# A delta-rule attention with masked copies of its diagonal blocks, a shorter norm, and the first batch of the following FFT mixing begun inside the attention's last steps

## What is computed

```python
# batch 4, 8 heads, 768 tokens, head size 48
k_n = k / (np.linalg.norm(k, axis=-1, keepdims=True) + 1e-06)
for t in range(S):
    y[:, :, t] = einsum('bhd,bhde->bhe', q[:, :, t], state)
    v_old = einsum('bhde,bhd->bhe', state, k_n[:, :, t])
    state = state + bt * einsum('bhd,bhe->bhde', k_n[:, :, t], v[:, :, t] - v_old)

# mixing, on x of 4 x 768 x 384 (the heads side by side)
mixed = np.real(np.fft.fft(np.fft.fft(x, axis=1), axis=2))
u = x + mixed
un = (u - mean(u)) / np.sqrt(var(u) + 1e-06)
x = u + np.maximum(un @ w_ch1, 0.0) @ w_ch2
```

## Time and profile before

| | |
|---|---|
| median of 3 runs | 904.81 us (901.88 to 904.92) |
| profiled execution, own time | 899.3 us |
| its span | 897.5 us |
| TensorE busy | 834.6 us (93%) |
| VectorE busy | 475.1 us (53%) |
| ScalarE busy | 301.3 us (34%) |
| GpSimd busy | 199.4 us (22%) |
| chain that ended last: TensorE, issue, VectorE, ScalarE | 61%, 20%, 11%, 4% |

### The profile page before, as it was taken

One profiled execution on the slowest core, in us unless ns is written; L12 is line 12 of the kernel. 1 busy time (PEld: TensorE's weight loads), 2 busy tenths in 40 slices (PEclk: granted clock), 3 DMA queues, 4 the chain that ended last, 5 costly groups with the idle time before them and its releaser, 6 DMA issues.

```text
span 897.5 us, 24703 instructions
## 1 busy us (share of the span) xinstructions
PE 834.6 (93%) x10634; PEld 809.9 (90%) x10634; DVE 475.1 (53%) x1092; ACT 301.3 (34%) x654; POOL 199.4 (22%) x167
## 2 busy tenths in 40 slices
PE   7368999999984999999999999999999999999998
PEld 6368989899884999999999999999899899899898
DVE  5999999999295554435443443333632432432421
ACT  4246575675431221122111211123441431431421
POOL 3123123023001803600540000000132222222231
PEclk9758779697886999999999999999999999999999
DMA  6633454422564030012000103003410010000001
GB/s 198 163 121 99 148 148 119 132 58 74 158 215 131 3 123 19 18 54 70 18 18 14 56 18 116 20 15 105 152 53 27 27 53 27 26 0 27 27 1 53
DMA packets 38074, 65.14 MB, mean 73 GB/s; under 512 B 4249, under 2 KB 26082, under 8 KB 37986
## 3 DMA queue, kind: packets, MB, share of 16 engines
q1 hardware_dynamic: 37986, 63.85, 22.7%
HBM read 46.86 MB, written 14.16 MB: 68 GB/s over the span
## 4 chain that ended last, share of the span: by engine, by line
PE 61%; issue 20%; DVE 11%; ACT 4%; POOL 2%; DMA 1%; SPq 1%; POOLq 0%; ACTq 0%; DVEq 0%
PE m_ps_h L1111 13%; PE g_ps_v L1622 11%; PE m_ps_d L1111 11%; PE ps_ga L423 4%; PE g_ps_y L1622 3%; PE g_ps_u L1622 3%; PE ps_y L509 3%; PE ps_y L514 2%; PE ps_u L492 2%; DVE t_lane L603 2%; DVE prod L599 2%; PE ps_r L474 2%; ACT tt L346 2%; PE ps_s L527 2%; POOL g_vn_lo L1519 2%
## 5 line engine op out<-in xcount | busy, mean ns | idle before, releaser
L1111 PE MATMUL m_ps_h<-m_unt_hi,m_w_hi 128*128 128x256 f32 x432 | 122.7, 284 | 2.1 <-DVE m_unt_lo L1301 2.1
L1111 PE MATMUL m_ps_h<-m_unt_lo,m_w_hi 128*128 128x256 f32 x432 | 121.9, 282 | 0.0
L1111 PE MATMUL m_ps_h<-m_unt_hi,m_w_lo 128*128 128x256 f32 x432 | 121.8, 282 | 0.0
L1307 DVE SCALAR_TENSOR_TENSOR m_h_lo<-m_ps_h,m_h_hi 128x512 fp32r<-128x512 f32 x72 | 49.8, 692 | 107.8 <-ACT m_h_hi L1011 107.8
L1111 PE MATMUL m_ps_d<-m_w_hi,m_h_hi 128*128 128x384 f32 x288 | 97.6, 339 | 0.0
L1111 PE MATMUL m_ps_d<-m_w_hi,m_h_lo 128*128 128x384 f32 x288 | 96.4, 335 | 0.0
L1111 PE MATMUL m_ps_d<-m_w_lo,m_h_hi 128*128 128x384 f32 x288 | 96.3, 334 | 0.0
L1011 ACT ACTIVATE m_h_hi<-m_ps_h 128x512 fp32r<-128x512 f32 x72 | 43.1, 598 | 151.0 <-PE m_ps_h L1111 151.0
L1111 PEld LDWEIGHTS m_ps_h<-m_unt_hi,m_w_hi 128*128 128x128 f32 x432 | 82.4, 191 | 2.6 <-DVE m_unt_lo L1301 2.5
L1111 PEld LDWEIGHTS m_ps_h<-m_unt_hi,m_w_lo 128*128 128x128 f32 x432 | 83.5, 193 | 0.0
L1111 PEld LDWEIGHTS m_ps_h<-m_unt_lo,m_w_hi 128*128 128x128 f32 x432 | 82.5, 191 | 0.0
(11 more groups left out here) (220 smaller groups left out, 1963.5 us busy)
## 6 DMA issues: line engine op xcount, KB each, us to landing
kq<-kq_g SPq DMA_DIRECT2D x48, 256.0 KB, 3.6
v_in<-v_g SPq DMA_DIRECT2D x12, 384.0 KB, 4.2
k_in<-k_g SPq DMA_DIRECT2D x12, 384.0 KB, 3.6
x_scr<-y_sb SPq DMA_DIRECT2D x24, 192.0 KB, 2.9
stage<-w_ch SPq DMA_DIRECT2D x6, 768.0 KB, 4.8
x_scr<-m_x_sb SPq DMA_DIRECT2D x24, 192.0 KB, 1.9
g_x<-x_scr SPq DMA_DIRECT2D x24, 192.0 KB, 4.5
out<-g_y SPq DMA_DIRECT2D x24, 192.0 KB, 1.9
```

The costliest lines, as they stand in the source:

```text
L1111: last = pe.matmul(out, first[x], second[y], start=(k == 0 and m == 0), stop=(k == n - 1 and m == 2))
L1307: dve.scalar_tensor_tensor(h_lo[:, 2 * g:2 * g + 2].rearrange("p f t -> p (f t)"), ps_h[g % 2][:, :], 0.0, h_hi[:, 2 * g:2 * g + 2].rearra ...
```

## The change

In the attention:

- `kmax` is gone; the root takes the diagonal of `g_lane` itself, with scale 0.25 and a small bias, so it is half the norm, and the Newton step then takes two operations where it took three. The last product of `lanes` is written straight into the diagonal of `t_lane`, which saves a copy; scaling `g_lane` now waits for it.
- `corners(g, c)` copies for one half of the units on all 128 partitions, twice, each time multiplied by a column of `half` that is 1 on the partitions wanted and 0 on the others. So `tt` needs no clearing at the start. Half c = 0 comes before the group, half c = 1 in its step 1, and `ps_u` waits only for the half it uses. Group 0 is now ordered like the others.
- The four Gram pieces of a group move by one step: from n = 4 to 7 to n = 5, 6, 7 and, for the last, step 0 of the next group (`gram_at`). Fetching them (`diagonal`) moves with them.
- The Gram pieces of group 2 wait until count 46 of group 0's chain.

In the mixing:

- The half of the first batch's spectrum that needs only early rows is multiplied inside the attention: cosines in step 5 and sines in step 6 of the last group. The sums lie in the banks `ps_e`, `ps_o` and `ps_d` until the second half is added.
- The early pieces of `x_tok` are loaded in steps 3 and 4 of the last group, the late ones straight from `y_sb`, not from DRAM.
- Chunk 2 of the weights is rounded on ScalarE, its remainder taken after `spectrum`; chunks 3, 4 and 5 have their remainders taken in `hidden(0, 0)`, behind g = 0, 2 and 4 (before: chunk 3 in `split` ahead of the spectrum, chunk 4 behind `norm`, chunk 5 behind g = 2).

```diff
+    def gram_at(i, n):
+        if n >= 5 and i + 3 < G:
+            return i + 3, n - 5
+        return (i + 2, 3) if n == 0 and i and i + 2 < G else None
...
             def roots(g):
-                act.wait_ge(kmax_ok, g + 1)
-                act.activation(root[:], kmax[:, g % 2], ACT.Sqrt).then_inc(root_ok, 1)
+                act.wait_ge(glane_ok, g + 1)
+                act.activation(root[:], ksum(g), ACT.Sqrt, bias=tiny[:, 0:1], scale=0.25).then_inc(root_ok, 1)
...
-                for a in (2 * h, 2 * h + 1):
-                    last = act.activation(tt[g % 2][quarter(a), :, H * (a % 2):H * (a % 2) + H], t_cols[quarter(a)],
-                                          ACT.Copy)
+                for a in range(2):
+                    last = act.activation(tt[g % 2][:, us, H * a:H * a + H], t_cols[:, us], ACT.Identity,
+                                          scale=half[:, a:a + 1])
                 last.then_inc(corner_ok, 1)
...
                 if 0 < i < G - 1 and n == 0:
                     solved_x(i, 0)
-                    corners(i, 1)
...
-                if 0 < i < G - 1 and n == 1:
+                if i < G - 1 and n == 1:
                     solved_w(i, 1)
+                    corners(i, 1)
...
             for what, g in FIRST:
+                if (what, g) == ("g", 2):
+                    pe.wait_ge(chain, WARM)
...
                     if m % NB == 0:
-                        pe.wait_ge(corner_ok, 2 * (g + 1))
+                        pe.wait_ge(corner_ok, 2 * g + c + 1)
...
+                for products in ahead.get(k - N * (G - 1), ()):
+                    products(pe)
...
-                dve.tensor_tensor(quot[:], ksum(g), rinv[:], ALU.mult).then_inc(newton, 1)
+                dve.scalar_tensor_tensor(quot[:], ksum(g), 0.25, rinv[:], ALU.mult, ALU.mult).then_inc(newton, 1)
                 link(2)
-                dve.tensor_tensor(quot[:], quot[:], root[:], ALU.add).then_inc(newton, 1)
+                dve.scalar_tensor_tensor(norm_l[:], quot[:], 1e-6, root[:], ALU.add, ALU.add).then_inc(newton, 1)
                 link(3)
-                dve.tensor_scalar(norm_l[:], quot[:], 0.5, 1e-6, ALU.mult, ALU.add).then_inc(newton, 1)
...
+        def residual_ahead(sp, first, last):
+            sp.wait_ge(att["ga_done"], att["pieces"] - 1)
+            rows = x_scr[0].rearrange("(m o) d -> o m d", o=2)
+            for part, t, k in early[first:last]:
+                m = k // 2
+                sp.dma_start(x_tok[part, t], rows[k % 2, m:m + part.stop - part.start]).then_inc(xt_in, 16)
...
+        def first_spectrum(pe, q, even, odd, n):
+            x, tab, m = (x_sin, ts_sb, MS) if q else (x_cos, tc_sb, MC)
+            pe.wait_ge(tab_in, 32)
+            pe.wait_ge(sin_ok if q else cos_ok, n + 1)
+            for ps, tiles in ((odd, (1, 3)), (even, (0, 2))):
+                for c in range(2):
+                    last = pe.matmul(ps[0:m, NK * c:NK * c + NK], x[:, c, tiles[n]], tab[:, tiles[n]],
+                                     start=(n == 0 and c == 0), stop=(n == 1), skip_group_check=True)
...
-                    if first and g == 2:
-                        weights(WC - 1)
+                    if first and g % 2 == 0:
+                        weights(DT + g // 2)
...
-            split(DT)
             spectrum(0, 0, ps_e, True)
-            spectrum(0, 1, ps_h[0], True)
+            spectrum(0, 1, ps_d[0], True)
+            weights(DT - 1)
             sums(0, 0)
             mirror(0, 0)
             norm(0, 0)
-            weights(NS)
```

More of the change, by code:

```diff
@@ L98, in attention @@
         beta = sb("beta", [P, G, H])
-        kmax = sb("kmax", [P, 2, H])
+        half = sb("half", [P, 2])
+        tiny = sb("tiny", [P, 1])
         root, rinv, quot, norm_l, rn, scale = (
@@ L260, in clear @@
                 pool.memset(t_lane[:], 0.0).then_inc(tl_zero, 1)
+            pool.memset(tiny[:], TINY / 4).then_inc(half_ok, 1)
+            pool.memset(half[:], 0.0).then_inc(half_ok, 1)
+            pool.wait_ge(half_ok, 2)
+            for a in range(4):
+                pool.memset(half[quarter(a), a % 2:a % 2 + 1], 1.0).then_inc(half_ok, 1)
+            pool.wait_ge(half_ok, 6)
             pool.memset(tri[:], 1.0).then_inc(tri_ok, 1)
@@ L276, in gpsimd @@
                                pattern=[[-1, P]], channel_multiplier=1).then_inc(ident_ok, 1)
-            for p in range(2):
-                pool.memset(tt[p][:], 0.0).then_inc(tt_zero, 1)
-            pool.wait_ge(tt_zero, 2)
             pool.wait_ge(ident_ok, 2)
@@ L534, in tensor @@
                     piece("a", i + 1, n - 2)
-                if n >= 4 and i + 3 < G:
-                    piece("g", i + 3, n - 4)
-                if i and n == 1:
+                if gram_at(i, n):
+                    piece("g", *gram_at(i, n))
+                if n == 1:
                     couple_w(i, 1)
-                if i and n == 2:
+                if n == 2:
                     couple_x(i, 1)
@@ L631, in last_inverse @@
                 dve.wait_ge(u_done, N * (g - 1))
-                for a in range(4):
-                    part = dve.tensor_copy(tt[g % 2][quarter(a), :, H * (a % 2):H * (a % 2) + H], t_cols[quarter(a)])
-                    if a % 2:
-                        part.then_inc(corner_ok, 1)
                 for c in range(2):
                     us = slice(HU * c, HU * c + HU)
+                    for a in range(2):
+                        part = dve.tensor_scalar(tt[g % 2][:, us, H * a:H * a + H], t_cols[:, us], half[:, a:a + 1], None,
+                                                 ALU.mult)
+                    part.then_inc(corner_ok, 1)
                     m = turn["w", g, c]
@@ L680, in upward @@
 def upward(tile, S):
+    end = S // 2 + P
     pieces = []
     for part, k, step in tokens(tile, S):
-        pieces.append((part, k if k < S // 2 else S + S // 2 - 1 - k))
+        row = k if k < S // 2 else S + S // 2 - 1 - k
+        n = (end - row + 1) // 2
+        if S // 2 <= row < end and part.start + n < part.stop:
+            pieces += [(slice(part.start, part.start + n), row), (slice(part.start + n, part.stop), row + 2 * n)]
+        else:
+            pieces.append((part, row))
     return pieces
@@ L872, in weights_ahead @@
             load_weights(sp, c)
+        first_tokens = [(part, t, k) for t in range(TT) for part, k in upward(t, S)]
+        late = [piece for piece in first_tokens if HS <= piece[2] < HS + P]
+        early = [piece for piece in first_tokens if piece not in late]
+        def residual_ahead(sp, first, last):
[4 more added lines that the diff above has]
+                sp.dma_start(x_tok[part, t], rows[k % 2, m:m + part.stop - part.start]).then_inc(xt_in, 16)
         ahead = {-2: (tables_ahead,), -1: (lambda sp: tokens_ahead(sp, 0, 3),), 0: (lambda sp: tokens_ahead(sp, 3, XE - 2),),
-                 1: (lambda sp: tokens_ahead(sp, XE - 2, XE),)}
-        for c in range(NS):
-            ahead[2 + c] = (lambda sp, c=c: weights_ahead(sp, c),)
+                 1: (lambda sp: tokens_ahead(sp, XE - 2, XE),), 2: (lambda sp: weights_ahead(sp, 0),),
+                 3: (lambda sp: weights_ahead(sp, 1), lambda sp: residual_ahead(sp, 0, len(early) // 2)),
+                 4: (lambda sp: weights_ahead(sp, 2), lambda sp: residual_ahead(sp, len(early) // 2, len(early)))}
         def first_batch(sp, results):
@@ L882, in first_batch @@
             sp.dma_start(x_in_sb[0:ROWS[3], 1, 3], results[0:P:2]).then_inc(x_in, 16)
+            for part, t, k in late:
+                sp.dma_start(x_tok[part, t], results[k - HS:P:2]).then_inc(xt_in, 16)
+            weights_ahead(sp, DT)
         def later_weights(sp):
@@ L1040, in batch @@
                     ahead["hi"](act, 0, ahead["split"])
+            act.wait_ge(att["ga_done"], att["pieces"])
+            act.wait_ge(att["corner_ok"], 2 * last_group + 2)
+            act.wait_ge(w_lo, DT - 1)
+            weights(DT - 1)
             odd_part(0, 0, ps_o, True)
-            odd_part(0, 1, ps_h[1], True)
+            odd_part(0, 1, ps_d[1], True)
+            act.wait_ge(att["y_done"], att["steps"])
+            weights(DT)
             for q in att["y_out"]:
@@ L1188, in first_weights_split @@
                 dve.wait_ge(att["corner_ok"], 2 * last_group + 2)
-                for c in range(DT):
+                for c in range(DT - 1):
                     split(c)
```

114 lines of the change are left out of this document (55 added, 59 removed).

## The result

| | before | after |
|---|---|---|
| median | 904.03 us (899.17 to 905.65) | 895.3 us (892.17 to 900.33) |
| profiled execution, own time | 899.3 us | 894.69 us |
| its span | 897.5 us | 892.9 us |

The ratio of the two is 0.992, with a 95% interval of 0.9899 to 0.9942: faster by 0.8%, 7 us, where 16.5 had been forecast; the median lies 2.3 us above the forecast's 884 to 893, within the wider range of 879 to 896.

A forecast was written before the change was run, and what follows sets the result against it. Bounds: VectorE's chain of inverses and the recurrence on TensorE and ScalarE in the attention, then the first batch's late residual. 11.5 + 6.5 - 1.5 = 16.5 us off 904.8 gave 888.3; forecast 884 to 893, wider range 879 to 896.

The forecast's parts named there:

- The norms: VectorE's chain in the attention: dropping kmax, a Newton operation and a copy saves about 0.1 us a group, 0.5 in group 0.
- The chain's floor: VectorE's chain of inverses: t_rows of group 5 starts at 214.7 us if no chain is held up.
- The recurrence: Group 2 on TensorE and ScalarE: 1152 matmuls, 31.9 us, plus 2 for the passage, 34 us where it took 40.2.
- the passage: Change from one attention group to the next, where TensorE waited and its clock fell: 2 us put on top of the matmuls.
- The attention: Whole attention: the copy of w_sb and corner copies of group 5 done at 220.2 for 231.7, a gain of 11.5 us.
- The root in group 2: ScalarE's queue, step 4 of group 2: the root must wait for `to_lanes` of chain 3, counted as 1.5 us.
- Group 0's early start: Start of the attention: group 0 begins about 5 us earlier, which buys nothing since group 1 waits for its t_rows.
- The first batch: Start of the mixing: sums end near 273.3 and `mirror` starts at 273.5 for 280.1, a gain of 6.5 us.
- what it adds behind: Three remainders in `hidden(0, 0)` may wait for GpSimd: 1.5 us lost, between 0 and 5.
- the clock falls at every passage: Rival, chance 0.17: groups 1 to 3 take 38 us each, attention gains only 5, total 893 to 897.

The follow-up runs named there:

- spread: Changed kernel with both halves of v issued in step 0 and two late quarters of the queries moved to steps 4 and 6: 894.61 us, ratio 0.991.
- att_paced: New attention with the old mixing, at most 640 KB of transfers under way in steps 8 to 37: 897.82 us, ratio 0.9953 to the kernel before.
- mix_only: Mixing of the changed kernel with the attention of the one before, products in steps 5 and 6 included: 897.9 us, ratio 0.994.
- att_only: Attention of the changed kernel with the mixing of the one before: 903.14 us, ratio 0.9987.
- bare: Changed kernel with most loads of keys, queries, v and diagonal blocks of later groups cut, so not computing the result: 884.84 us, ratio 0.9797.
- after_light: Changed kernel loading keys and queries of groups 4 and 5 for 8 of 128 partitions only, so not computing the result: 889.06 us, ratio 0.984.
- gram_old: Changed kernel with the Gram pieces back in steps 4 to 7 and the diagonal blocks fetched in step 0: 894.94 us, ratio 0.9908.
- paced: Changed kernel with at most 640 KB of transfers under way from step 8 to step 47: 903.5 us, ratio 1.0011.
- paced_late: Changed kernel with at most 640 KB under way in steps 8 to 47 and the early residual pieces issued late: 898.31 us, ratio 0.9972.

## Why the prediction was half right

- **The norms** (0.1 us a group): right. A chain takes 33.9 us for 34.1, and the column and `scale` took over the wait for GpSimd.
- **The chain's floor** (t_rows of group 5 at 214.7): right as a floor, 215.3 without the transfers. In the changed kernel it was 219.0, since v and the diagonal blocks of later groups come in step with the recurrence, and the diagonal blocks a step later than before.
- **The recurrence** (34 us for group 2): this is the step that failed. I counted 1152 matmuls at 27.7 ns, 31.9 us, with the clock up, and 2 us for the passage. Group 2 took 40.0 us: 34.6 busy, since the clock was 0.91, and 5.4 idle, of which four waits for TensorE's own instructions are 5.2. These waits stood in no term of the sum. The price of a matmul was right (32.15 us for 1156 at the full clock), and quiet packets alone would have allowed the 34: 9.2 of them at 3.5 to 3.8 us are 32 to 35. But behind a backlog one took up to 6.4, and the clock fell behind most of the waits. Group 2 took 37.3 to 39.0 us in the runs of the new attention with fewer or reordered transfers in the groups or with 640 KB at most under way, and in none of them 34. Group 1 took 38.8 us as before, so w_sb of group 2 came at 122.4 and not at 118. Before, TensorE needed 5.2 us for 126 matmuls wherever it ran at 40.9 ns, and most packets came behind that unseen.
- **The attention** (11.5 us): 1.2 alone (between -1.5 and 3.9), about 9 with the transfers cut in both kernels. Cutting them was worth 11 us to the changed kernel and 4 to the one before, so some 7 us of the attention (4 either way) went to what the transfers do: late packets with the clock's falls behind them, and a late v and late diagonal blocks. How it splits between these is not shown. `spread` took the late v away and half of the packet waits, and gained nothing that can be told; `att_paced` gained 3 us, within the noise, and paced both.
- **The root in group 2** (1.5 us): it never came to wait, since the recurrence was not early enough; it ran at 149.8.
- **Group 0's early start**: bought nothing, as said (w_sb of group 1 at 83.56 for 82.75).
- **The first batch** (6.5) and **what it adds behind** (1.5): right together, 5.4 us for 5.0 in `mix_only`, where `mirror` comes 6.7 us sooner behind the first u of group 5 (34.1 us for 40.8). In the changed kernel it is 3.2 (37.6), as steps 40 to 47 took 29.1 us for 24.1; the waits for packets there are about as long in both (2.7 and 2.4 us). `mix_only` has 25.7 and `att_only` 26.2 there; and `bare`, `after_light`, `spread` and `gram_old`, whose last group has the same order as the changed kernel's, have 26.9 to 27.3. So about 3 of the 5 us come with the change, and the other 2 are this one trace's. From `hidden` on, 1.1 us were lost.
- **The rivals.** The number lies in the range of "the clock falls at every passage" (893 to 897), and the mechanism was that rival's in part only. The clock was higher in groups 1 and 2 than before, 0.85 and 0.91 for 0.78 and 0.83, and the time did not follow; but it did not stay up, and it fell behind waits for packets, also where no passage was. That the total came out in this rival's range is luck. None of my rivals named TensorE's own instructions. The 20% of `issue` in the table of before was no warning of it: most of it lies behind 290 us, and up to there it is 4.7% of the chain (7.6% up to 284 us now).

Open remains what holds group 2 at 37.8 us. In `bare` it is the clock (35.7 us busy, 2.1 idle), whose two falls in this group, from 122.5 and 139.6 on, begin 1.1 and 0.8 us behind such waits of 0.6 and 1.3 us; in `after_light` it is the waits (32.2 busy, 5.6 idle), and no run takes both away. Single traces of one kernel differ in this as well (0.77 and 1.00 for group 4 in `paced` and `paced_late`, whose programs are the same up to there).

## What to carry to other kernels

A stretch of many small matmuls has a floor that is not in the price of a matmul: count its instructions, divide them by 256, and multiply with the time from packet to packet that the trace shows (3.5 to 3.8 us here, quiet). Price the waits above this floor too: here they grew from 3 to 13 us, as much as the change had won elsewhere in the attention (5.9 us of busy time and 4.4 of waits for the corner copies). Look for gaps named "issue" in the middle of equal, ready matmuls, and count the matmuls between them. Holding back transfers may help a little (1 to 3 us with 640 KB under way in the attention, within the noise, and nothing in the old kernel), but 512 KB or the wrong stretch cost 8 to 10 us against the changed kernel.

## What the hardware showed beyond this

- TensorE stood still in the middle of equal, ready matmuls, for up to 2.5 us, at multiples of 126 matmuls with their weight loads, where the packet of 256 instructions was late; the profile shows the wait as "issue".
- In the changed kernel, six of seven falls of the clock between 85 and 222 us began 0.5 to 1.3 us behind such a wait.
- A full clock did not by itself make a group faster: 37.8 us at 1.00 with 5.6 us of waits (`after_light`), and 37.8 at 0.86 with 2.1 idle and fewer transfers (`bare`).
- 127 added waits for a count long reached were 63 instructions on TensorE, and moved the borders by 30 or 31 matmuls.
